# The first head's preparation divided between ScalarE and VectorE in an attention and mixture-of-experts kernel

## What is computed

```python
# q, k, v: [2, 8, 1152, 64], float32
q_pool = q.reshape(B, H, S // 2, 2, D).mean(axis=3)          # 576 queries a head
scores = q_pool @ k.transpose(0, 1, 3, 2) / sqrt(D)
attn = softmax(scores)                                        # with + 1e-9 in the denominator
x = attn @ v                                                  # -> [1152, 512]
x = moe_top2(x, w_gate, w_noise, noise, w1, w2)               # 8 experts, hidden size 1024
h = x @ w_in;  out = (h * cos(h)) @ w_out                     # hidden size 2048
```

## Time and profile before

| | |
|---|---|
| median of 3 runs | 867.7 us (865.75 to 868.94) |
| profiled execution | 867.97 us, of which the profile's span is 866.2 us |
| mean granted TensorE clock | 0.998 |
| TensorE busy | 845.9 us, 98% of the span |
| VectorE busy | 493.7 us, 57% |
| ScalarE busy | 421.9 us, 49% |
| GpSimd busy | 401.3 us, 46% |

### The profile page before, as it was taken

One profiled execution on the slowest core, in us unless ns is written; L12 is line 12 of the kernel. 1 busy time (PEld: TensorE's weight loads), 2 busy tenths in 40 slices (PEclk: granted clock), 3 DMA queues, 4 the chain that ended last, 5 costly groups with the idle time before them and its releaser, 6 DMA issues.

```text
span 866.2 us, 15441 instructions
## 1 busy us (share of the span) xinstructions
PE 845.9 (98%) x4894; PEld 751.0 (87%) x4895; DVE 493.7 (57%) x983; ACT 421.9 (49%) x775; POOL 401.3 (46%) x293
## 2 busy tenths in 40 slices
PE   7999999999999989999999999999988999999998
PEld 6899999999999887888888888888877889999897
DVE  6788778887778886323232323232234776575664
ACT  3777777777777763211121112111134565565544
POOL 8554445546787006567959956859022030000000
PEclk9999999999999999999999999999999999999999
DMA  5212111152251017986536636445225020100101
GB/s 133 63 42 79 46 41 41 41 159 63 89 165 49 1 56 236 339 296 222 171 111 219 201 133 194 133 147 181 73 84 183 1 73 1 37 1 0 38 1 37
DMA packets 51377, 90.50 MB, mean 104 GB/s; under 512 B 9360, under 2 KB 18576, under 8 KB 50832
## 3 DMA queue, kind: packets, MB, share of 16 engines
q1 hardware_dynamic: 40688, 66.47, 23.2%
q10 hardware_dynamic: 7296, 12.59, 4.5%
q0 software_dynamic: 3360, 11.01, 4.2%
HBM read 73.00 MB, written 17.06 MB: 104 GB/s over the span
## 4 chain that ended last, share of the span: by engine, by line
PE 88%; DVE 5%; ACT 2%; POOL 2%; issue 1%; DMA 1%; another core or an unknown queue 0%; DVEq 0%; POOLq 0%; ACTq 0%
PE ps L1583 10%; PE ps L1585 10%; PE ps L1584 10%; PE ps L1405 5%; PE ps L1435 4%; PE ps L1451 4%; PE ps L1453 4%; PE ps L1452 4%; PE ps L1436 4%; PE ps L1684 3%; PE ps L1683 3%; PE ps L1682 3%; PE ps L1667 3%; PE ps L1669 3%; PE ps L1668 3%; PE ps L1622 2%
## 5 line engine op out<-in xcount | busy, mean ns | idle before, releaser
L623 POOL TENSOR_TENSOR W<-stage,W 128x2048 fp32r<-128x2048 f32 x32 | 147.2, 4600 | 2.6
L999 DVE TENSOR_REDUCE mx<-ps 128x1 f32<-128x384 f32 x225 | 119.6, 551 | 18.2 <-PE ps L1405 18.2
L1011 DVE TENSOR_TENSOR pl__77<-ps,ph 128x576 fp32r<-128x576 f32 x144 | 108.0, 750 | 33.5 <-ACT ps L775 33.5
L770 ACT ACTIVATE ph<-ps 128x576 fp32r<-128x576 f32 x144 | 93.9, 652 | 53.4 <-PE ps L1436 52.4
L775 ACT ACTIVATE ps<-ps 128x576 f32<-128x576 f32 x144 | 93.5, 649 | 0.0
L844 ACT CAST hh<-ps 128x512 fp32r<-128x512 f32 x50 | 26.9, 590 | 129.4 <-PE ps L1622 125.9
L1451 PE MATMUL ps<-ph,vs 128*65 128x288 f32 x288 | 86.0, 299 | 0.4 <-ACT ot L729 0.4
L1435 PE MATMUL ps<-qat,kt 128*128 128x288 f32 x288 | 83.7, 306 | 1.3 <-ACT qbt L722 0.6
L1453 PE MATMUL ps<-ph,vs 128*65 128x288 f32 x288 | 84.8, 294 | 0.0
L1452 PE MATMUL ps<-pl__77,vs 128*65 128x288 f32 x288 | 84.6, 294 | 0.0
L1583 PE MATMUL ps<-W,hh 128*128 (+1 forms) x200 | 80.0, 400 | 1.8 <-DVE hl L1269 1.8
(11 more groups left out here) (210 smaller groups left out, 1966.6 us busy)
## 6 DMA issues: line engine op xcount, KB each, us to landing
stage<-in_moe_w_dram SPq DMA_DIRECT2D x32, 1024.0 KB
y_slots<-ys ACTq DMA_DIRECT2D x25, 256.0 KB
x_slots<-ring SPq DMA_DIRECT2D x22, 256.0 KB
xs<-x_slots ACTq DMA_DIRECT2D x22, 256.0 KB
kn<-in_k_dram SPq DMA_DIRECT2D x16, 288.0 KB, 3.3
vn<-in_v_dram SPq DMA_DIRECT2D x16, 288.0 KB, 2.9
stage<-in_moe_w_in_dram SPq DMA_DIRECT2D x4, 1024.0 KB
stage<-in_moe_w_out_dram SPq DMA_DIRECT2D x4, 1024.0 KB
```

Of the source, the lines that this page charges most:

```text
L623: pl.tensor_tensor(W[:, slot, 1, part], stage[:, j % 2, :], W[:, slot, 0, part].bitcast(F32), ALU.subtract).then_inc(w_ready, 1)
L999: ve.tensor_reduce(mx3[:, i:i + 1], ps[:, bank_of(hh, ("m", i)), 0:PIECE], AX_X, ALU.max).then_inc(m_ev, 1)
L1011: ve.tensor_tensor(pl_[:, j % 3, :].rearrange("p (a n) -> p a n", a=2), ps[:, 2 * s_par(hh, j):2 * s_par(hh, j) + 2, 0:HQ], ph[:, j % 3, : ...
```

## The change

Only head 0's preparation and one group of head 1 are touched:

- ScalarE makes the high part of the keys and the second of the two copies of `qp`; VectorE keeps the first copy and the two low parts.
- VectorE copies out head 0's `("k", 3)` group, the 512-column part of head 0's `qbt`, and head 1's `("k", 3)` group; ScalarE leaves these out.
- VectorE's copy of the identity into `turner`, the small fill and the negation of `tok` move from behind the five reductions to ahead of the keys' low part, with their waits. `low_pad` becomes the last fill and now stands behind the copy of `("k", 3)`.
- The load of the tail of head 0's queries is issued by ScalarE's queue instead of SyncE's, ahead of the table load.
- TensorE waits for `FILLS` instead of `FILLS - 2` ahead of `qb_group(0, 0, 0)`.

```diff
--- before.py
+++ after.py
@@ SyncE
             sp.dma_start(kn[:, 0, :, :].rearrange("p j d -> p (j d)"),
                          k_v[0:1].rearrange("o p n -> (o p) n")).then_inc(k_in0, 16)
-            sp.dma_start(qn[0:QTAIL, 0, QC - 1, :, :].rearrange("p t d -> p (t d)"),
-                         q_v[0:1, (QC - 1) * P:SQ, :].rearrange("o p n -> (o p) n")).then_inc(q_in0, 16)
@@ ScalarE
-            def cycle(p, hh, main, prep, before, ahead=True, early=False):
+            def cycle(p, hh, main, prep, before, ahead=True, early=False, queries=True):
...
-                            if prep and kind == "k":
+                            if prep and kind == "k" and queries:
                                 kq_move(p, hh, slot, bank_of(hh, slot))
...
+            act.dma_start(qn[0:QTAIL, 0, QC - 1, :, :].rearrange("p t d -> p (t d)"),
+                          q_v[0:1, (QC - 1) * P:SQ, :].rearrange("o p n -> (o p) n")).then_inc(q_in0, 16)
             sc.preload_act_table_set("natural_log_exp_and_others")
-            for slot in (("n", 0), ("n", 1), TAIL, ("k", 3)):
+            act.wait_ge(k_in[0], 16)
+            sc.copy(ks[:, 0, :, 0, :].bitcast(F32R), kn[:, 0, :, :]).then_inc(kh_done, 1)
+            act.wait_ge(qp_done, 1)
+            sc.copy(qa[:, :, 1, :].bitcast(F32R), qp[:, :, :]).then_inc(qa_done, 1)
+            for slot in (("n", 0), ("n", 1), TAIL):
                 kq_move(0, 0, slot, FIRST_BANK[slot])
             kq_move(0, 1, ("n", 0), 0)
             kq_move(0, 1, ("n", 1), 1)
-            qb_move(0, 0, 0)
             qb_move(0, 0, 1)
             kq_move(0, 1, TAIL, bank_of(0, ("q", 1)))
             act.wait_ge(zeroed, FILLS)
-            cycle(0, 1, True, True, False, early=True)
+            cycle(0, 1, True, True, False, early=True, queries=False)
@@ VectorE
-            dve.wait_ge(zeroed, FILLS - 3)
-            dve.wait_ge(k_in[0], 16)
-            ve.tensor_copy(ks[:, 0, :, 0, :].bitcast(F32R), kn[:, 0, :, :]).then_inc(kh_done, 1)
+            dve.wait_ge(consts_done, 9)
+            ve.tensor_copy(turner[:, :, 0:D + 1],
+                           ident[0:D + 1, 0:D + 1].unsqueeze(1).to_broadcast([D + 1, NHEAD, D + 1])).then_inc(zeroed, 1)
+            ve.memset(tok[QTAIL:P, QC - 1:RT:QC], 0.0).then_inc(zeroed, 1)
+            dve.wait_ge(zeroed, FILLS - 1)
+            ve.tensor_scalar(minus_tok[:, :], tok[:, :], -1.0, None, ALU.mult).then_inc(minus_done, 1)
             dve.wait_ge(kh_done, 1)
             ve.tensor_tensor(ks[:, 0, :, 1, :], kn[:, 0, :, :], ks[:, 0, :, 0, :], ALU.subtract).then_inc(kl_done, 1)
             dve.wait_ge(q_in[0], 32)
             ve.tensor_tensor(qp[:, :, :], qn[:, 0, :, 0, :], qn[:, 0, :, 1, :], ALU.add).then_inc(qp_done, 1)
             dve.wait_ge(qp_done, 1)
-            for n in range(2):
-                ve.tensor_copy(qa[:, :, n, :].bitcast(F32R), qp[:, :, :]).then_inc(qa_done, 1)
+            ve.tensor_copy(qa[:, :, 0, :].bitcast(F32R), qp[:, :, :]).then_inc(qa_done, 1)
             dve.wait_ge(qa_done, 2)
             dve.wait_ge(kl_done, 1)
             ve.tensor_tensor(qb[:, 0, :, 0:D], qp[:, :, :], qa[:, :, 0, :], ALU.subtract).then_inc(kq_ready, 1)
+
+            def queries_move(h, at):
+
+                dve.wait_ge(kq_done, 4 * (h + 1))
+                ve.tensor_copy(qat[:, h % 2, 0:4 * P], ps[:, at, :]).then_inc(kq_ev, 1)
+
+            queries_move(0, FIRST_BANK["k", 3])
             ve.memset(low_pad, 0.0).then_inc(zeroed, 1)
...
-            dve.wait_ge(zeroed, FILLS - 2)
+            dve.wait_ge(zeroed, FILLS)
             for c in range(QC):
...
-            dve.wait_ge(consts_done, 9)
-            ve.tensor_copy(turner[:, :, 0:D + 1],
-                           ident[0:D + 1, 0:D + 1].unsqueeze(1).to_broadcast([D + 1, NHEAD, D + 1])).then_inc(zeroed, 1)
-
-            ve.memset(tok[QTAIL:P, QC - 1:RT:QC], 0.0).then_inc(zeroed, 1)
-            dve.wait_ge(zeroed, FILLS)
-            ve.tensor_scalar(minus_tok[:, :], tok[:, :], -1.0, None, ALU.mult).then_inc(minus_done, 1)
+            dve.wait_ge(qb_done, 1)
+            ve.tensor_copy(qbt[:, 0, 0:4 * P], ps[:, bank_of(0, ("q", 0)), :]).then_inc(qb_ev, 1)
+            queries_move(1, bank_of(1, ("k", 3)))
             cycle(0, 1, True, True, False)
@@ TensorE
-            pe.wait_ge(zeroed, FILLS - 2)
+            pe.wait_ge(zeroed, FILLS)
             qb_group(0, 0, 0)
```

## The result

| | before | after |
|---|---|---|
| median of 22 runs each | 867.25 us (865.75 to 869.77) | 869.43 us (865.79 to 870.97) |
| ratio | | 1.0021, 95% interval 1.0012 to 1.0029 |
| profiled execution / its span | 867.97 / 866.2 us | 867.81 / 866.1 us |
| first score matmul of head 0 | 8.68 us | 11.44 us |
| head 0's first scores for the exponentials | 17.70 us | 20.41 us |

What follows compares the result with a forecast made beforehand. TensorE, 88% of the chain, was taken to bound the kernel, with prologue delays arriving whole. +2.6 - 0.4 = +2.2 us on 867.97 gave 870.2, less 0.3 for the median: 869.9 us, range 865.8 to 872.3.

Steps and rivals of the forecast that it cites:

- rival (a): Prologue: GpSimd's fills hold nothing on VectorE, so only the gains are left, 867.3 us; chance 0.26.
- Rival (b): Prologue: only GpSimd's first fill holds, the negation slips in before the second; low half +0.85 us, 868.2 us; chance 0.08.
- parts 3 and 4: Head 0's query copies side by side, transposed-query copy moved to VectorE: about -0.2 us at the score matmuls.
- The low half, +2.6 us: Head 0's keys on VectorE: low half starts near 7.6 us, after copy and negation waited for GpSimd's fills; +2.6 us.
- TensorE's pace, taken as 0 in the sum: Prologue matmuls: no slowdown in the sum; one low-clock stretch, at most 1.7 us, only in the range's upper end.
- The argument against it: Against a falling clock: from 15 to 20 us TensorE was idle 1.76 of 5 us, granted clock still 1.00.
- the sign that I named: TensorE's granted clock between 8 and 15 us was to show whether the clock falls.
- Rival (c): TensorE's clock falls after the late low half, half pace from 8.4 to about 15 us: +3.4 us, 873.3 us; chance 0.06.
- Part 2: Query-load tail moved to ScalarE's queue, later SyncE loads issued 0.6 us earlier: 0 to +0.5 us, taken as 0.
- Parts 5 and 6: Low-half copy at 16.80 us and head 1's copy at 19.12 us moved to VectorE: -0.1 and -0.05 us.
- 1 for 1: Before 20 us: a microsecond won or lost in the prologue arrives whole at the kernel's end.
- A wrong side reason: Prologue: VectorE's f32r casts ran unstretched beside GpSimd's fills, taken as not of the excluding kind.

Runs made afterwards that it cites:

- place_only: The kernel before with only the identity copy, token fill and negation moved ahead of the keys' high half; 870.78 us, ratio 1.0032.
- negation_back: The changed kernel with only the negation put back, behind the low-half query copy; 869.94 us, ratio 1.0013 to the kernel before.
- tail_on_sync: As place_back, but with the tail of the query load issued by SyncE again; 868.23 us, ratio 1.0006 to the kernel before.
- rounded_out: The changed kernel with identity copy and negation writing f32r instead of f32; 871.02 us, ratio 1.0025 to the kernel before.
- fills_in_eighths: The changed kernel with each of GpSimd's two k1 fills cut into eight pieces; 868.19 us, ratio 1.0005 to the kernel before.
- longer_filler: The changed kernel with 11 instead of 7 filler matmuls ahead of TensorE's first key wait; 869.09 us, ratio 1.0013 to the kernel before.
- after_again: The changed kernel once more, with nothing altered; one run, 872.24 us.
- place_back: The changed kernel with identity copy and token fill back behind the reductions, negation behind the low-half query copy; 867.7 us, ratio 0.9995 to the kernel before.
- on_scalar: The changed kernel with identity copy and negation made by ScalarE, query tail load issued by SyncE; 867.62 us, ratio 0.9984 to the kernel before.

## Why the prediction was right, and where its steps were not

The forecast was 869.9 us and +2.2 us; measured are 869.43 us and, from the ratio, +1.8 us (1.0 to 2.5). The mechanism, that the moved copy and negation wait for GpSimd's fills one after the other, came out nearly to the tenth (copy over 2 us, second fill stretched, negation ending with it), and rival (a), that a fill holds nothing, is dead. Rival (b) too. But that the sum is so close is in good part luck: two of its terms missed in opposite directions, by 1.0 and by 1.4 us. Up to the first score matmul the trace adds up to +1.63 (start of the transposes) - 0.29 (parts 3 and 4) + 1.42 (pace) = +2.76 us, where the prediction had +2.6 - 0.2.

- **The low half, +2.6 us: mis-sized, it was +1.6.** I let the low half start when the negation had ended. It ran while the negation waited: `place_only` shows the cast behind it ending at 7.36 with it, `negation_back` shows the share of each instruction (0.5 and 1.1 us). TensorE's transposes began at 7.44 instead of 8.4.
- **TensorE's pace, taken as 0 in the sum, cost about 1.4 us.** From the start of the transposes to the first scores it takes 4.00 us in the changed kernel, 2.58 in `tail_on_sync` at full pace. I put the low clock among the rivals and in the upper end of the range, at 1.7 us for one stretch. The half pace was there in both profiles of the changed kernel, in `rounded_out`, `negation_back` and `fills_in_eighths`. The argument against it, idle time with a granted clock of 1.00 from 15 to 20 us, holds for that stretch, where transposes last 272 ns, but does not carry over to the first microseconds, and the sign that I named, the granted clock between 8 and 15 us, can't show it. The changed kernel's window from 8 to 9 us (length, busy, granted clock) reads 1.00, and so does the next, while its transposes start 0.21 us apart (9.20, 9.41) and each lasts (min/median/max ns) as long as a filler matmul of the first 5 us:

```profile
8.00:9.00 1.00, 1.00 (x7) 1.00 0.88 56
...
L1531 PE MATMUL ps<-ident x14: 421/421/579, 2.0 to 5.0; 128*128 128x128 f32 x14
...
L1404 PE MATMUL ps<-ident,ks x8: 421/421/475, 7.4 to 9.0; 128*128 128x128 f32 x8
```

  In the prologue, before its first recorded change, that column can't be relied on; the length of a known form of matmul can (272 ns in the kernel before from about 6 us; 421 ns in `place_only` from 9.8 us, where the column does read 0.50). `longer_filler` and `after_again` show how much the pace varies, 1.2 us less and 1.4 us more than in the first profile. Rival (c) was alive: in `after_again` head 1's first score matmul stands at 23.94, 4.1 us late, of which 1.6 are the low half and -0.4 the gains, so that the pace makes up 2.9 against the 3.4 of the rival; that run took 872.24 us. In `place_only`, worked out in the same way, it makes up 1.8. What decides how long the half pace lasts stays open.
- **Parts 3 and 4, -0.2 us: right.** From the start of the transposes to the first scores it took 2.87 us before and 2.58 in `tail_on_sync`, -0.29. In the changed kernel TensorE did not wait for the query copies either: they were ready at 7.93, and it came to them at 9.41.
- **Part 2, 0 us: mis-sized where it shows.** Issued behind the rest of the query load on ScalarE's queue and with head 1's loads closer behind (the two were not tried apart), its tail costs 0.29 us in `place_back`. In the changed kernel the sum stood behind the late low half anyway, as said.
- **Parts 5 and 6, -0.15 us: right.** From the first scores (11.44) to head 1's maxima (22.48) it takes 11.04 us instead of 11.16.
- **1 for 1 up to the end: shown up to 310 us.** In the changed kernel the lag is +2.64 at head 1's maxima and +2.7 at 310 us; in `fills_in_eighths` +0.66 and +0.8, in `longer_filler` +1.43 and +1.5, in `on_scalar` -0.60 and -0.5. Behind that the profiles scatter by more than a microsecond at 326 to 335 and at 657 us, and the measured +1.8 doesn't exclude that a part is given back there. That stays open.
- **A part of the +1.8 may be the clock.** Of the changed kernel's 22 runs, seven with a mean granted clock of 1.000 have a median of 867.8 us, six with 0.992 to 0.994 one of 869.7 (869.4 to 871.0). Of the 83 runs of the kernel before that went with the experiments, one had so low a clock. So a part of the difference may come with low-clock stretches, which the changed kernel seems to have more often; `place_only`'s profile (0.992) shows such stretches from 9 to 16 us and again from 26. How large a part is not shown: the clocks of the 22 runs of the kernel before are not on record.
- **A wrong side reason:** casts to f32r are not of a harmless kind, as I had them for rival (a); `rounded_out` shows it. And one reading was loose: of the pair behind the reductions only the negation was stretched to the other's end; L608 ended 0.99 us behind the copy's end (17.59 against 16.60), as it had its own work still to do.

## What to carry to other kernels

Before moving an SBUF-to-SBUF copy or a one-source operation on VectorE into an idle stretch, look at what GpSimd does there: a ten-column negation cost over a microsecond because it had to wait for a fill. Look for such a pair in the trace first, one instruction longer than its kind and ending with one of the other engine's; cutting GpSimd's instruction into pieces or giving the VectorE one to ScalarE removes it. Neither was faster than the kernel before by more than the noise. And price a stall of TensorE's feeder with the pace at which TensorE comes back: in the two profiles of the changed kernel that added 1.4 and 2.9 us.

## What the runs showed of the hardware beyond what was expected

- A GpSimd fill, which reads nothing, shuts out the VectorE copy and tensor_scalar of this case until it ends (2.38 against 0.69 us, 1.83 against 0.17), and is shut out by the copy (2.45 against 2.02; a piece of a fill 0.89 against 0.33). The cast of the keys beside a fill is not (0.75 us). Of this the prediction had only the Trainium skill ("SBUF — State Buffer", "Who interferes with whom"); the measurement agrees.
- The VectorE instructions behind a waiting one do their work meanwhile and end with it: a cast of 0.75 us, begun at 5.61, ended at 7.36 with the negation that had begun at 5.53 (`place_only`); in the changed kernel two did, the low half at 7.36 and the sum at 7.37. One that waits for a semaphore of the held one waits on: in `place_only` the low half begins only at 7.42.
- TensorE begins this program at half pace, with a granted clock recorded as 1.00: the filler matmuls of 128 columns last 421 ns each up to 5.4 us, as the transposes, of the same form, do in `place_only` at a granted clock of 0.50, and 272 ns from about 6 us on in the kernel before. The changed kernel, with 2.04 us of idle time in between, is still at 421 ns until about 10.6 us, and in one execution at half pace until about 16.8. The Trainium skill, "TensorE: Matmul & The Clock Gate", Part 1, says that the default state is the slow one and that activity releases it, from a point that varies from run to run; these rows agree, with a spread wider than the page gives.
